# Pauses between the second mixture's scatters, an earlier mark, and a longer table of due chunks

## What is computed

```python
# 1. a causal convolution with 7 taps, softmaxed, 8 heads of 24 channels
out = np.einsum('hk,bskhg->bshg', w, x_unf)
# 2. a mixture of 8 experts, one expert to a token
expert_idx = np.argmax(x @ w_gate, axis=1)
out[mask] = gate_w[mask, None] * (np.maximum(x[mask] @ w1[e], 0) @ w2[e])
# 3. a second mixture of 8 experts, two to a token, chosen from noisy logits
noisy_logits = x @ w_gate2 + np.log1p(np.exp(x @ w_noise)) * noise
top2 = np.argpartition(-noisy_logits, 2, axis=1)[:, :2]
out[mask] += top2_w[mask, k, None] * (h @ w2_2[e])
```

## Time and profile before

| | |
|---|---|
| median of 3 runs | 1995.59 us (1994.42 to 1995.81) |
| the profiled execution | 1985.47 us |
| its span | 1983.5 us |
| PE busy | 1886.2 us, 95% |
| DVE, ACT, POOL busy | 64%, 46%, 47% |
| mean granted clock of TensorE | 0.98 |

### The profile page before, as it was taken

The page is one execution under the profiler, slowest core; times in us unless marked ns, Lnnn a source line. Parts: engine busy times, 40 slices in busy tenths (PEclk is TensorE's granted clock), DMA queues, the critical chain, the costliest instruction groups (busy, mean ns, idle before and its releaser), DMA issues.

```text
span 1983.5 us, 50949 instructions
## 1 busy us (share of the span) xinstructions
PE 1886.2 (95%) x14103; PEld 1832.6 (92%) x14104; DVE 1274.3 (64%) x4251; ACT 914.4 (46%) x2425; POOL 929.5 (47%) x1301
## 2 busy tenths in 40 slices
PE   7986689999999999799999999999999999999998
PEld 5666689999999999799999999999999999999998
DVE  4675378787887788755555655655655655655555
ACT  4553145455555555434444444444444444445444
POOL 3777734343334333444444444444444444444444
PEclk9997799999999999999999999999999999999999
DMA  6644232332332323232231221322322322222221
GB/s 215 233 149 136 79 108 86 116 120 84 113 101 93 117 87 109 81 97 63 64 99 61 66 92 61 100 66 63 101 63 67 97 61 65 96 62 87 78 62 48
DMA packets 114007, 185.92 MB, mean 94 GB/s; under 512 B 21580, under 2 KB 89924, under 8 KB 111808
## 3 DMA queue, kind: packets, MB, share of 16 engines
q1 hardware_dynamic: 73392, 104.86, 17.5%
q0 software_dynamic: 40320, 79.90, 11.9%
q10 hardware_dynamic: 272, 0.92, 0.1%
HBM read 112.10 MB, written 77.61 MB: 96 GB/s over the span
## 4 chain that ended last, share of the span: by engine, by line
PE 83%; DVE 5%; issue 5%; POOL 4%; another core or an unknown queue 1%; DMA 1%; DVEq 1%; ACT 1%; ACTq 0%; SPq 0%; POOLq 0%
PE bank L1145 26%; PE bank L1146 12%; PE bank L1126 8%; PE bank L1129 8%; PE bank L1128 8%; PE bank L1130 8%; PE bank L1127 7%; POOL rows_of_mixture L1229 3%; PE bank L1115 2%; PE bank L996 2%; DVE h_l L843 1%; PE bank L1063 1%; PE bank L1116 1%; POOL pause L1231 1%
## 5 line engine op out<-in xcount | busy, mean ns | idle before, releaser
L1145 PE MATMUL bank<-w2hl,h_h 128*128 128x384 f32 (+1 forms) x2832 | 867.9, 371 | 10.5 <-DVE w2hl L669 3.6
L1146 PE MATMUL bank<-w2hl,h_l 128*128 128x192 f32 (+1 forms) x2832 | 722.9, 255 | 0.0
L843 DVE SCALAR_TENSOR_TENSOR h_l<-bank,h_h 128x512 fp32r<-128x512 f32 x708 | 477.9, 689 | 177.6 <-ACT h_h L557 90.7
L557 ACT ACTIVATE h_h<-bank 128x512 fp32r<-128x512 f32 x708 | 422.4, 597 | 357.4 <-PE bank L1130 316.0
L1145 PEld LDWEIGHTS bank<-w2hl,h_h 128*128 128x128 f32 x2832 | 536.1, 189 | 17.2 <-issue 10.0
L1146 PEld LDWEIGHTS bank<-w2hl,h_l 128*128 128x128 f32 x2832 | 545.1, 192 | 0.0
L1126 PE MATMUL bank<-x_h,w1mh 128*128 128x256 f32 x1416 | 403.4, 285 | 16.9 <-issue 8.9
L1256 POOL DMA_INDIRECT rows_of_mixture<-x_in,pos x248 | 245.9, 992 | 363.3 <-DVE h_l L843 173.3
L1128 PE MATMUL bank<-x_h,w1ml 128*128 128x256 f32 x1416 | 401.0, 283 | 2.2 <-issue 2.2
L1129 PE MATMUL bank<-x_h,w1lh 128*128 128x256 f32 x1416 | 401.8, 284 | 0.8 <-issue 0.8
L1130 PE MATMUL bank<-x_h,w1ll 128*128 128x256 f32 x1416 | 400.0, 282 | 1.1 <-issue 1.1
(11 more groups left out here) (193 smaller groups left out, 1895.9 us busy)
## 6 DMA issues: line engine op xcount, KB each, us to landing
rows<-rows_of_mixture SPq DMA_DIRECT2D x179, 208.0 KB
raw<-in_w_of_both SPq DMA_DIRECT2D x17, 1024.0 KB
raw<-in_w_of_both SPq DMA_DIRECT2D x17, 768.0 KB
x_in<-in_x SPq DMA_DIRECT2D x16, 768.0 KB
out<-zeros SPq DMA_DIRECT2D x61, 192.0 KB
raw<-in_moe_w_turned SPq DMA_DIRECT2D x8, 768.0 KB
rows_of_mixture<-pad_rows SPq DMA_DIRECT2D x21, 208.0 KB, 10.2
rows_of_mixture<-x_in,pos POOLq DMA_INDIRECT x248
```

What stands on the lines that cost most here:

```text
L557: nc.scalar.activation(h_h[:, 2 * p:2 * p + 2, :].rearrange("p c t -> p (c t)"), bank[1 + p][:], ACT.Relu).then_inc(hh_ready[m], 1)
L843: V.scalar_tensor_tensor(h_l[:, 2 * p:2 * p + 2, :].rearrange("p c t -> p (c t)"), bank[1 + p][:], 0.0, h_h[:, 2 * p:2 * p + 2, :].rearran ...
L1145: T.matmul(dst, h_h[:, c, tok], both, start=(c == 0), stop=False)
L1146: last = T.matmul(bank[5 + a][:, 0:width], h_l[:, c, tok], w2hl[:, c, 0:width], start=False, stop=(c == F // P - 1))
```

## The change

Three things are changed. Behind three of the four sends of `store_rows`, all but the last, comes the memset `pause` and a wait for it, against a register that holds the count. `mark_landed(c - 1)` moves from behind the eighth send of chunk c to behind the fourth. The table has an entry for each chunk from 4 to 14 and the last one twice, 12 columns for 4, so `due` can be any whole number from 4 to 14, or 16.

```diff
-EARLY_AT = [XROW + 2 * k for k in range(4)]
+EARLY_AT = list(range(4, CHUNKS - 1))
+DUE_COLUMNS = len(EARLY_AT) + 1
+MARK_AT = 3
...
-                    v = sp_.value_load(due[0:1, bass.ds(j, 1)], min_val=EARLY_AT[0], max_val=CHUNKS)
+                    v = sp_.value_load(due[0:1, bass.ds(j, 1)], min_val=CHUNKS - DUE_COLUMNS, max_val=CHUNKS)
...
                     V.tensor_copy(first_count[:, k:k + 1], bank[2][0:1, RANKS:RANKS + 1])
+                    if c == EARLY_AT[-1]:
+                        link(V.tensor_copy(first_count[:, k + 1:k + 2], bank[2][0:1, RANKS:RANKS + 1]))
...
-                shape = [1, len(EARLY_AT), E]
+                shape = [1, DUE_COLUMNS, E]
...
-                V.tensor_scalar(due[:], slots_in[:], -2.0, float(CHUNKS), ALU.mult, ALU.add).then_inc(due_ready, 1)
+                V.tensor_scalar(due[:], slots_in[:], -1.0, float(CHUNKS), ALU.mult, ALU.add).then_inc(due_ready, 1)
...
                     link(G.memset(pause[:], 0.0))
-                if c > 0:
-                    mark_landed(c - 1)
+                    if t == MARK_AT and c > 0:
+                        mark_landed(c - 1)
...
                                              oob_is_err=False).then_inc(scattered2[r % 2], 16)
+                        if (k, a) != (1, 1):
+                            G.memset(pause[:], 0.0).then_inc(paused, 1)
+                            until((paused, s * 3 + (CHUNKS * CHUNK + 2 * k + a + 1)))
```

More of the change, by code:

```diff
@@ L146, in attention_and_two_mixtures @@
         slots_in = sb("slots_in", [1, E])
-        first_count = sb("first_count", [1, len(EARLY_AT)])
+        first_count = sb("first_count", [1, DUE_COLUMNS])
         slot_full = sb("slot_full", [1, E])
-        slot_in = sb("slot_in", [1, len(EARLY_AT), E])
+        slot_in = sb("slot_in", [1, DUE_COLUMNS, E])
         late = sb("late", [1, 1], i32)
@@ L678, in _ @@
             C_STEPS = 11
+            LAST_COPY = EARLY_AT[-1]
             full = [TILE, CHUNK, E]
@@ L733, in place_first @@
                 V.scalar_tensor_tensor(c_pos[:, c % XROW, :], c_best[:], -float(CAP), c_posf[:], ALU.mult, ALU.add).then_inc(pos_ready, 1)
-                assert link.n == C_STEPS, link.n
+                assert link.n == C_STEPS + (c == LAST_COPY), link.n
             def early_slots():
                 link = Steps(dve, dve_due)
-                shape = [1, len(EARLY_AT), E]
+                shape = [1, DUE_COLUMNS, E]
                 link(V.tensor_scalar(slot_full[:], expert[0:1, :], float(SLOT), float(SLOT), ALU.mult, ALU.add))
@@ L755, in _ @@
             for c in range(1, CHUNKS):
-                link = Steps(dve, dve_c, C_STEPS * c)
+                link = Steps(dve, dve_c, C_STEPS * c + (c > LAST_COPY))
                 choose_first(c, link)
```

## The result

| first comparison | median, us | ratio to before |
|---|---|---|
| before, 11 runs | 1995.96 (1994.36 to 1997.65) | |
| after, 11 runs | 2001.79 (1997.35 to 2009.97) | 1.0033 [1.0023, 1.0043] |
| after, the profiled execution | 2001.59, span 1999.5 | |

The change costs 5.8 us. 1983.0 had been predicted, with a range up to 1998.0. The profiled execution of after is at its median; that of before was 10 us under its own, so the two traces differ by more (16 us) than the medians.

What follows compares the result with a forecast made beforehand. PE, busy 95%, was taken as the bound, losing time where unpaused send trains starve sequencers. -10.84 - 3.05 + 0.65 + 0.6 = -12.6 us took 1995.59 to 1983.0 us; range 1975 to 1998.

Steps and rivals of the forecast that it cites:

- The pauses' term: Pauses between the second mixture's sends remove PE's 10.84 us stall after the front stage and DVE's 3.05 us between mixtures.
- hand-over: End of first mixture: pauses make POOL's second fetch of so_far late, leaving PE 0 to 3 us short; 0.6 taken.
- 2.06: Predicted us from send to send within a paused turn: 0.98 + 0.22 + 0.86, the last for the start behind the wait.
- The argument from the slow register instructions to the sends: After the front stage, SP's register instructions took 697 ns for 203; long trains of unpaused sends were taken to starve sequencers.
- Its premise that all sequencers were slow together: In PE's 10.84 us loss after the front stage, no operand was missing; sequencers of all engines were slow together.
- the mark's 0.65 us: Front stage: a mark costs 0.65 us between two sends, the same in mid-chunk; the last chunk lands 0.65 us later.
- That slot 5 waits for all 16 chunks: Earlier marks load slots 3 and 4 5.8 us earlier, but slot 5 moves by +0.65: gain 0, cost 0.65.
- since the front stage is the nearest case with the same instruction and the same pause, and shows none: Reason for taking the whole gain of both stalls: front-stage sends, paused and 1.44 us apart, show no such stall.
- The stall isn't the sends': Rival: the stall belongs to profile recording or something that fell into 239 to 254; only costs left, 1997 us, chance 0.18.
- The pauses stretch the train: Rival: dense sends starve sequencers despite pauses, so the train after the front stage lasts longer; 2012 us, chance 0.12.
- The table: Seven more entries of 0.15 us on DVE and one duplicate, beside POOL: cost 0, gain 0.
- Slots 3 and 4: First mixture: their loads come 5.8 us earlier, at about 186.6 and 211, only moving PE's idle time to before slot 5.

Runs made afterwards that it cites:

- full groups: Three of five groups of runs, each on another chip, where the kernel before ran at 1968 us and every trace held 25,559 to 25,805 semaphore events.
- thinned: Conditions of the first comparison and the last two groups: the kernel before ran at 1985 to 1996 us, traces held only 16,261 to 17,237 semaphore events.
- the run with the mark at the chunk's end: Changed kernel without any pause in the front stage, mark back behind the eighth send: 2040.88 us, 1.0236 of before.

## Why the prediction was wrong, by its own steps

**The pauses' term was right in its conditions, its parts less so.** -10.84 - 3.05 + 0.6 = -13.3 us for pauses and hand-over; the pauses alone measured -13.8 (1971.44 - 1985.22). Put beside before's trace, that of the pauses alone starts the last layer 2 matmul of the first mixture 12.8 us earlier (817.12 for 829.96; 10.84 were forecast) and the first layer 1 matmul of the second a further 3.2 us (3.05). Then it gives back 1.9 us: 1.0 in that layer 1, which it does at a granted clock of 0.65 against 0.76, and 0.9 before layer 2 of slot 1 (0.6). So the size of the sum is partly luck. The sends came 2.20 us apart for 2.06, since behind the new pause POOL is idle for 1.00 us, not 0.86. The stretch from 244 to 254 is full, and the gap between x_l and x_h on DVE at the second mixture's start is gone. The argument from the slow register instructions to the sends was sound as far as that the rate of sends decides. Its premise that all sequencers were slow together holds in one respect and not in another. SP's first slow instruction starts at 239.6, and PE goes on without a gap until 243.9, at the end with a matmul each 0.12 us. Once they are slow, though, they move in common steps of 0.7 us: SP's instructions start at 239.6, 240.3, 241.0, 241.7 and so on, POOL's sequencer starts one at 240.3 and one at 241.7, and PE's restarts lie in the same steps. L284 on SP's sequencer and then the timeline of PE, both before:

```profile
L284 SPq MOVE out<-zeros x1: 689/689/689, 240.3 to 240.3; - x1
```

```profile
245.31 0.28 PE L1128 MATMUL bank<-x_h,w1ml 128*128 128x256 f32 x1 [1.13 <-issue]
246.03 0.28 PE L1129 MATMUL bank<-x_h,w1lh 128*128 128x256 f32 x1 [0.45 <-issue]
```

A rival that the prediction passed over, late loads of instructions, can be read from before's trace: such loads have queues of their own on the page, q8 and q14, and from 239 to 254 neither moved anything. The DMA queues of that window (packets, MB, share):

```profile
q0 software_dynamic: 528, 1.17, 21.5%
q1 hardware_dynamic: 688, 0.62, 13.9%
```

**A term with the wrong sign: the mark's 0.65 us, "and I take the same in mid-chunk".** It costs 0.03 there. At the chunk's end the next send came 0.78 us after the memset; in mid-chunk after 0.17. Nor is it the place alone: with no mark there, the send that opens a chunk follows the last one by 1.45 us like any other. Only the two together cost 0.65. Where 0.65 stood behind each of 14 chunks and now 0.03 stands in 15, the last send is to come 8.7 us earlier, and came 7.2 to 7.9 us earlier in the full groups. That slot 5 waits for all 16 chunks, so that the earlier places of the marks gain nothing, was right, and had the wrong number in it: +0.65 us instead of -7. In the full conditions this is most of the gain: where before and the changed kernel ran side by side, the last send came 7.9 us earlier and the time was 9.1 us less.

**The step that failed, and turned the sign: "since the front stage is the nearest case with the same instruction and the same pause, and shows none".** It was taken for a proof that pauses suffice, when it was one point, at one send in 1.525 us with a break every eighth. At 1.45 us the front stage starved (PE busy 80.25 of 100 us), and gave back more than the pauses had won. The sum had no term for it. The parts were costed alone; one part's stall and another's rate were the same resource. Before's own front stage was already touched, with 551 matmuls from 30 to 130 where its full trace has 574, which could not be seen without that trace; but the waits for "remote" and the missing landings of the sends were there.

**The rivals.** "The stall isn't the sends'" was half right: in the full conditions the pauses gave 1.0005. "The pauses stretch the train" was wrong: they didn't lengthen the stall in any run. None of the cases had the loss in the front stage, so the 0.12 for slower was given to a mechanism that wasn't there.

**The table**: 0, and at most 0.2%. **Slots 3 and 4**: forecast for 186.6 and 211; in the starved trace they came at 239.55 and 249.57, in the full one at 178.59 and 201.76, since the marks before them cost less.

**What stays open** is what makes a comparison thinned. The runs come with a granted clock for each, so nothing here shows an execution without any recording. The Trainium skill ("NOTIFIC — the notification-queue block", 7.1 Overflow) says that a full record queue drops or overwrites records, or stalls the producer. The thinned traces would fit both kinds, with a third of the events missing and sequencers that step each 0.7 us (SP and POOL both start one at 240.3 in before), but they show no queue, and something else that holds up all sequencers would look the same. The steps of 0.7 us that several sequencers share point at something common to them; a slow path of one engine alone doesn't make them. Each group ran on another chip, and whether it is the chip, its host or the recording was not tried.

## What to carry to other kernels

Before a part of an edit is costed alone, ask which rate it raises: an edit that removes a break from a train of sends is an edit of the same kind as removing the pauses. A stage that "shows no stall" is one point at its own rate; give its distance to the stage that does show one. And look at whether the trace is complete (landings present, few releasers "remote"): the same kernel stood at 0.982 and at 1.023 of before, so a version is chosen for the conditions it will run in. Of the versions run in both kinds none beats before in both: the pauses alone are the safe one (0.9927, and 1.0005 where there is nothing to gain), and without front pauses it is the fastest seen (1933.38 us) and the worst.

## What the runs showed of the hardware that was not expected

- The start of a send behind a one-element memset took 0.17 us within a chunk and 0.78 us behind the chunk's end, where POOL waits for the next chunk's semaphores too. The same mark cost 0.03 us or 0.65 us, and the chunk's end without it nothing.
- In the thinned conditions DVE started up to 3.8 us after the matmul it waits for with POOL's indirect sends every 1.45 us, and up to 13.1 us with one every 1.25 us (the run with the mark at the chunk's end), both at some chunks only; in the full ones it was 0.03 to 0.05 us at any rate down to 1.25 us, from the second chunk to the fifteenth.
- In the stall after the front stage SP's, POOL's and PE's sequencers went on in common steps of 0.7 us, with no load of instructions under way.
- A third of the semaphore events of a trace can be missing (16,297 of 25,687 for the same kernel) with all 50,949 instructions in it, and where that was so, the kernel was 17 to 28 us slower.
